# First expert weights in three loads, first x issued by ScalarE, gated lo parts behind the first split, block ends without the GpSimd drain

## The reference

```python
# 1. gated linear attention, B, H, S, D = 4, 8, 768, 48
for t in range(S):
    state = f[:, :, t, :, None] * state + einsum('bhd,bhe->bhde', k[:, :, t], v[:, :, t])
    y[:, :, t] = einsum('bhd,bhde->bhe', q[:, :, t], state)
# 2. mixture, one expert of 8 per token; 3072 tokens of 384, w1 384 x 1024, w2 1024 x 384
logits = x @ w_gate + modality_bias[modality_id]
e_idx = argmax(logits, axis=1)
for e in range(E):
    h = maximum(x[e_idx == e] @ w1[e], 0.0)
    out[e_idx == e] = gate_w[e_idx == e, None] * (h @ w2[e])
# 3. gated layer on all tokens, d_ff 1536
xn = x / sqrt(mean(x * x) + 1e-6) * rms_g
g, val = xn @ w_gate2, xn @ w_val
return (g * sigmoid(g) * val) @ w_out
```

## Time and profile before

| | us |
|---|---|
| median of three runs | 925.57 (925.3 to 928.85) |
| profiled execution | 919.33 |
| its span, first to last instruction | 917.6 |
| mean granted TensorE clock | 0.977 of full speed |
| PE busy | 859.9 (94%) |
| ACT busy | 389.6 (42%) |
| DVE busy | 474.4 (52%) |
| POOL busy | 158.0 (17%) |

### The profile page before, as it was taken

One profiled execution on the slowest core, in us unless ns is written; L12 is line 12 of the kernel. 1 busy time (PEld: TensorE's weight loads), 2 busy tenths in 40 slices (PEclk: granted clock), 3 DMA queues, 4 the chain that ended last, 5 costly groups with the idle time before them and its releaser, 6 DMA issues.

```text
span 917.6 us, 15619 instructions
## 1 busy us (share of the span) xinstructions
PE 859.9 (94%) x5512; PEld 785.4 (86%) x5512; DVE 474.4 (52%) x752; ACT 389.6 (42%) x765; POOL 158.0 (17%) x155
## 2 busy tenths in 40 slices
PE   7998898579889999999799999999999999999996
PEld 6887787579889999999688888888888888888885
DVE  5788888486666456657144433334333343333331
ACT  3788788245654455556132331232133123222121
POOL 6224542241115700000000020010010002001001
PEclk9899999879999999999899999999999999999999
DMA  8667662297666797775200010010020000000000
GB/s 163 130 125 155 164 146 78 84 340 274 223 213 216 237 357 243 258 239 193 86 1 1 2 68 1 1 69 0 0 69 0 0 0 34 0 0 34 0 0 34
DMA packets 33135, 97.23 MB, mean 106 GB/s; under 512 B 7888, under 2 KB 24272, under 8 KB 29648
## 3 DMA queue, kind: packets, MB, share of 16 engines
q1 hardware_dynamic: 29264, 87.38, 32.1%
q0 software_dynamic: 3840, 9.47, 2.8%
HBM read 76.75 MB, written 20.08 MB: 106 GB/s over the span
## 4 chain that ended last, share of the span: by engine, by line
PE 50%; POOL 0%; ACT 0%; DVE 0%; issue 0%; ACTq 0%; DVEq 0%
PE g_ps L1533 6%; PE g_ps L1534 6%; PE acc_ps L1532 5%; PE g_ps L1532 5%; PE acc_ps L1534 5%; PE acc_ps L1533 5%; PE v_ps L1534 5%; PE v_ps L1532 5%; PE v_ps L1533 5%; PE xT_ps L1527 1%; POOL out L1430 0%; ACT x_hi L1445 0%; DVE x_lo L1485 0%; DVE h_lo L1511 0%; DVE hid L1501 0%
## 5 line engine op out<-in xcount | busy, mean ns | idle before, releaser
L1498 DVE TENSOR_TENSOR gs<-g_ps,sig 128x512 f32<-128x512 f32 x72 | 49.8, 692 | 180.9 <-ACT sig L1455 180.9
L1455 ACT ACTIVATE sig<-g_ps 128x512 f32<-128x512 f32 x72 | 43.1, 598 | 176.3 <-PE g_ps L1534 176.3
L1466 ACT CAST h_hi<-hid 128x512 fp32r<-128x512 f32 x72 | 44.7, 620 | 149.6 <-DVE hid L1501 149.6
L1532 PE MATMUL acc_ps<-wo_hi,h_hi 128*128 128x384 f32 x288 | 98.5, 342 | 0.2 <-DVE h_lo L1511 0.2
L1534 PE MATMUL acc_ps<-wo_lo,h_hi 128*128 128x384 f32 x288 | 97.1, 337 | 0.0
L1533 PE MATMUL acc_ps<-wo_hi,h_lo 128*128 128x384 f32 x288 | 96.7, 336 | 0.0
L1277 DVE TENSOR_TENSOR w_lo<-w_in,w_hi 128x768 fp32r<-128x768 f32 x52 | 59.2, 1159 | 65.4 <-ACT w_hi L1168 65.2
L1308 PE MATMUL h_ps<-x_hi,w_hi 128*128 128x256 f32 x312 | 89.1, 285 | 2.6 <-DVE x_lo L1261 2.6
L1309 PE MATMUL h_ps<-x_hi,w_lo 128*128 128x256 f32 x312 | 89.0, 285 | 0.0
L1310 PE MATMUL h_ps<-x_lo,w_hi 128*128 128x256 f32 x312 | 88.9, 285 | 0.0
L1534 PE MATMUL g_ps<-x_lo,wg_hi 128*128 128x512 f32 x216 | 86.0, 398 | 0.0
(11 more groups left out here) (191 smaller groups left out, 1794.6 us busy)
## 6 DMA issues: line engine op xcount, KB each, us to landing
w_raw<-in_w SPq DMA_DIRECT2D x13, 1536.0 KB, 7.0
w_in<-in_w SPq DMA_DIRECT2D x13, 1536.0 KB, 7.6
qkf_in<-in_qkf SPq DMA_DIRECT2D x48, 288.0 KB, 5.0
x_regions<-zero_row SPq DMA_DIRECT2D x14, 384.0 KB, 6.6
x_group<-x_regions SPq DMA_DIRECT2D x13, 384.0 KB, 3.6
y_sorted<-x_group SPq DMA_DIRECT2D x13, 384.0 KB, 6.2
v_in<-in_v SPq DMA_DIRECT2D x24, 192.0 KB, 4.8
g_in<-in_wg SPq DMA_DIRECT2D x3, 768.0 KB, 5.1
```

The lines of the kernel that those rows point to most:

```text
L1455: nc.scalar.activation(sig[:], g_ps[:], ACT.Sigmoid).then_inc(sig_done, 1)
L1466: nc.scalar.copy(h_hi[:, fb % 2], hid[:]).then_inc(h_hi_done, 1)
L1498: nc.vector.tensor_tensor(gs[:], g_ps[:], sig[:], ALU.mult).then_inc(gs_done, 1)
L1532: nc.tensor.matmul(out, hi, rhs_hi, start=first, stop=False)
```

## The change

All four blocks are opened with `no_gpsimd_drain=True`: at a block's end POOL goes to the barrier without its DRAIN instruction. In the mixture w1 is loaded in three DMAs with a semaphore each, for every tile, and ACT waits for each third by itself. x of the first tile is no longer loaded by SP but by ACT, ahead of Exp. ACT and DVE take x in front of the last third of the first w1. POOL waits for the first tile's `x_split` and `w1_split` before the first of its gated lo parts. The warm-up has 24 matmuls instead of 48.

```diff
-        block = ctx.enter_context(nc.Block())
+        block = ctx.enter_context(nc.Block(no_gpsimd_drain=True))
...
-        w1_landed = sem("w1_landed")
+        w1_landed = [sem(f"w1_landed{k}") for k in range(KD)]
...
-            def load_w(e, src, dst, landed):
-                sp.dma_start(dst[:], src[e]).then_inc(landed, 16)
+            def load_w1(e):
+                for k in range(KD):
+                    sp.dma_start(w1_in[:, k * F1:(k + 1) * F1], w1[e][:, k * F1:(k + 1) * F1]).then_inc(w1_landed[k], 16)
+
+            def load_w2(e):
+                sp.dma_start(w2_in[:], w2[e]).then_inc(w2_landed, 16)
...
             pad(e0)
-            load_w(e0, w1, w1_in, w1_landed)
-            sp.wait_ge(scattered, 16 * B)
-            load_x(0)
-            load_w(e0, w2, w2_in, w2_landed)
+            load_w1(e0)
+            load_w2(e0)
             sp.wait_ge(x_landed, 16)
...
+            pool.wait_ge(x_split, 1)
+            pool.wait_ge(w1_split, 1)
             for i, (_, hi, lo) in enumerate(thirds):
                 pool.wait_ge(g_hi_done, i + 1)
...
-            def hi_w1(j):
-                act.wait_ge(w1_landed, j * 16 + 16)
-                for k in range(KD):
+            def hi_w1(j, parts=range(KD)):
+                for k in parts:
+                    act.wait_ge(w1_landed[k], j * 16 + 16)
...
             act.wait_ge(table_ready, 1)
+            row0 = act.value_load(table[0:1, FIRST:FIRST + 1], min_val=0, max_val=E * REGION - TM)
+            act.wait_ge(scattered, 16 * B)
+            act.wait_ge(padded, 16)
+            act.dma_start(x_in, x_regions[bass.ds(row0, TM), :].rearrange("(s p) d -> p s d", p=P)).then_inc(x_landed, 16)
             act.wait_ge(shifted, 1)
             nc.scalar.activation(prob, biased, ACT.Exp).then_inc(exp_ready, 1)
             nc.scalar.preload_act_table_set("sigmoid_and_others")
-            hi_w1(0)
+            hi_w1(0, range(KD - 1))
             hi_x(0)
+            hi_w1(0, range(KD - 1, KD))
...
             dve.wait_ge(table_ready, 1)
-            lo_w1(0)
+            lo_w1(0, range(KD - 1))
             lo_x(0)
+            lo_w1(0, range(KD - 1, KD))
...
-            for _ in range(WARM_UP):
+            for _ in range(WARM_UP // 2):
```

More of the change, by code:

```diff
@@ L1074, in body @@
                     sp.wait_ge(w1_split, j + 1)
-                    load_w(e, w1, w1_in, w1_landed)
+                    load_w1(e)
                     sp.wait_ge(w2_split, j * GR + GR)
-                    load_w(e, w2, w2_in, w2_landed)
+                    load_w2(e)
                     sp.wait_ge(x_landed, j * 16 + 32)
@@ L1250, in _, with lo_w1 @@
             nc.vector.reciprocal(of_token[:, :, 0], total[:]).then_inc(gate_ready, 1)
-            def lo_w1(j):
-                for k in range(KD):
+            def lo_w1(j, parts=range(KD)):
+                for k in parts:
                     dve.wait_ge(w1_hi_done, j * KD + k + 1)
@@ L1256, in lo_w1 @@
                                                    w1_hi[:, k].bitcast(F32), ALU.subtract)
-                last.then_inc(w1_split, 1)
+                if KD - 1 in parts:
+                    last.then_inc(w1_split, 1)
             def lo_x(j):
```

## The result

| | before | changed |
|---|---|---|
| median of 10 runs each, us | 925.43 (920.79 to 928.85) | 930.91 (926.89 to 934.66) |
| ratio, 95% interval | 1 | 1.0058 [1.0032, 1.0085] |
| profiled execution, us | 919.33 | 932.13 |
| its span | 917.6 | 930.4 |
| mean granted TensorE clock | 0.977 | 0.966 |

The changed kernel is 0.58% slower, 5.4 us. The forecast was 924.8 with a range up to 929.0; the time lies above both, within 0.5 us of rival 2's 930.4.

A forecast was written before the change was run, and what follows sets the result against it. TensorE, busy 859.9 of 917.6 us, was taken as the bound, so its idle places count. Terms -1.71 + 1.25 + 1.7 - 2.02 = -0.8 us gave a median of 924.8 us, range 920.2 to 929.0.

The forecast's parts named there:

- rival 2: Start of the mixture: x on ACT's queue lands behind all the weights, at 202.0; total 930.4 us; chance 0.08.
- I take the middle, 196.3: Start of the mixture: first tile's x, issued by ACT about 191.9, lands at 196.3, between 195.5 and 197.1.
- The start: From routing table to tile 0's first product: that product comes at about 200.3 instead of 202.32, -2.0 us.
- Behind POOL: Tile 0: SP's gated loads wait for POOL, delaying tile 1's x; PE idles 3.3 us, second product 1.25 later.
- The half clock in the first product: Tile 0: a clock fall there costs nothing up to the 3.3 us PE waits for tile 1's x anyway.
- the one behind the idle: Tile 0's second product: PE's new idle makes the clock fall, +1.7 us, between 0 and 3.4.
- Hidden behind SP's delay, and the next to show if that went: Tile 0: DVE's w2 beside POOL's subtractions is ready at 211.8, before tile 1's x has landed.
- rival 1: Tile 0: the wait on g_split doesn't decide, DVE does; no new clock fall; sum -5.0, 920.5 us; chance 0.16.
- The drains: Block ends: two of four POOL drains are on the path, -1.71 at the attention's end, -2.02 at the kernel's.
- Rival 3: Kernel's end: the last drain comes back behind the span, so -2.02 is lost; 926.8 us; chance 0.19.
- The pieces: Tile loop: w1 in pieces costs two more issues of 0.4 us per tile on SP, hidden; 0 effect.
- The sum: Whole kernel: drains, start with tile 0, and clock together give -0.8 us.

## Why the prediction was wrong

*The step that failed*: "I take the middle, 196.3, because w1 and w2 are now both issued ahead of it and share the engines". x landed at 201.8. Both ends of that bound, 195.5 and 197.1, were landings of x on SP's queue, with nothing of another queue beside it; neither holds what w2 on a second queue does. The turns were then 0.7 longer (1.54 for 0.82, at half clock), which the prediction had at nothing, and h0 came 20.0 behind T where 13.9 was forecast. Counted from T, the landing is 5.3 of these 6.1 us, the turns 0.7, the rest 0.1. The start is +4.1 instead of -2.0. With w2 moved away, x landed 5.8 us behind its issue and the start was at 16.2: shown. Rival 2 had the landing nearly right (202.0) for a reason that is not the right one, service behind w2; the packets show turns, in which x loses by the shortness of its rows, and a late first packet. I gave it 0.08. That its 930.4 is so near to the measured 930.9 is partly luck: by the profile's parts the start and tile 0 are 1.4 us worse than in it, and the parts add up to 0.9 more than the medians show.

*Behind POOL*: forecast 3.3 idle and 1.7 of clock, 5.0 for tile 0; measured 5.9, of it 3.48 of idle, 1.7 of clock behind it and 0.8 of longer half clock in the first product. x of tile 1 was issued 11.2 behind h0 (forecast 9.9): POOL's pair took 8.28 instead of 6.82, with DVE's three subtractions of w2 beside it, 5.11 us for the first two and 3.52 for the third (POOL's pair took 6.84 in the kernel without its waits, where DVE had w2's parts not yet to do; that the two hold each other up is inferred). The half clock in the first product took nothing from the time, as said, since x of tile 1 would have been no earlier, and the one behind the idle was 1.7, as said. Taking POOL's waits away gave 5.0 us, moving SP's loads 5.4. The step held, its size was 1 us short. "Hidden behind SP's delay, and the next to show if that went" held for DVE's w2 as well: with SP's loads moved, PE waits 0.7 and 2.0 us for it in the two kernels with an early first product. PE's wait of 3.48 for x of tile 1 refutes rival 1.

*The drains*: forecast -3.73; alone they gave -5.6 and -2.7, so the size holds within what two measurements tell. T itself doesn't show it: it lies between 184.7 and 188.2 over all profiles, with the attention's own spread. The stretches behind the last work do: from DVE's flag to T it is 11.50 us before and 9.3 to 9.8 in the thirteen profiles without the drains, and from POOL's last DMA to the end 4.07 and 2.0. That is 1.7 in the pair of before and changed and 2.1 at the end, 3.8 for a forecast of 3.73. Rival 3 is refuted: 1.73 us outside the span as before, and the last 2 us did go.

*The pieces*: forecast 0, and drains with pieces against drains alone shows no difference.

*The sum*: -3.7 + 4.1 + 5.9 = +6.3, measured +5.4. The single execution shows +12.8: besides the 6.3, 4.8 in tiles 1 to 6 and 1.85 of a later end of the attention. Tiles 5 and 6, with most of POOL's 24 small indirect DMAs in them, take 41.4 here, 41.6 when repeated, and 38.2 to 51.8 in the other kernels, and the median does not follow them: the drains alone had 44.4 and a ratio of 0.9939. The 38.0 of the kernel before are those of an execution 6 us below its median.

*What stays open*: what the whole warm-up is worth here; what delays x's first packet; why DVE's w_lo comes sooner in tiles 2 and 4 with w2 in three pieces; what stops the engines in tile 5 in four of the profiles, and whether it is the chip.

## What to carry to other kernels

Before moving a small load to another engine's queue, look at what the first queue holds at that moment and at the row lengths: the two queues here shared by packets, so short rows lost beside long ones, and a load that everybody waits for is better with nothing beside it that can wait (w2 behind x gave 3.8 us of the start). Before a wait is added to an engine, follow who waits for what it gives and what stands behind that waiter in its list: here SP's queue made POOL's delay 5 us, and once that was mended DVE's share of it came out, 0.7 to 2 us where the first product was early. Bounds for a transfer need rows with the same neighbours; where there are none, the far end is "behind all that is issued ahead", and that case deserves more than a small chance.

## What the runs showed of the hardware

- Two queues took turns by equal numbers of packets on the 16 engines: 33 to 30, 29 to 29, and 71 to 73 in a microsecond, with packets of 1,536 against 12,288 and 4,096 bytes.
- A load on ACT's queue behind weights already issued on SP's had its first packet after 1.7 to 4.0 us, where a load on an empty SP queue had it after 1.05. Without w2 ahead of it, the first packet came 8.2 to 8.6 us behind T on either queue, about when w1 ran out (eight kernels); with w2 ahead, 3.5 to 4.0 behind its issue (six).
- A DRAIN of POOL at the end of a block took 1.71 and 2.02 us on the path; without them the two stretches were 1.7 and 2.1 us shorter, and leaving out all four gave 2.7 and 5.6 us.
- Three VectorE subtractions of 128x768 took 0.96, 4.23 and 3.52 us beside two of GpSimd, where one takes 0.95 without; GpSimd's pair took 8.28 instead of 6.84.
- In the mixture's tile 5 all engines but POOL can stand still for "issue" while POOL issues indirect DMAs: 6.0 to 9.4 us of such waits of PE in the four profiles of the second chip, none in the ten others; tiles 5 and 6 took 46.0 to 51.8 us there and 38.0 to 44.4 elsewhere, with TensorE's clock at its lower level in part of them.
